# One core: a slot sort in two runs, a tile's x split by halves, and an expert loop turned by one step

## The chip, the cores and the metric

The kernel runs on one core of a Trainium2 chip. The metric is the device time of one execution in microseconds; lower is better. Matrix products run on TensorE (PE), elementwise work on VectorE (DVE) and ScalarE (ACT), indexed transfers are issued by GpSimd (POOL), the other transfers by SyncE (SP).

## What is computed

Three stages, each feeding the next:

```python
# 1: retention: state = gamma*state + k v^T ; y = scale * q state    (4 x 8 heads x 768 x 64)
# 2: dense, gated:
x = ((x @ w_a) * (x @ w_b)) @ w_out            # 3072 x 512, inner 1536
# 3: eight experts, one for each token:
logits = x @ w_gate
e_idx = np.argmax(logits, axis=1)
for e in range(8):
    mask = e_idx == e
    h = np.maximum(x[mask] @ w1[e], 0.0)       # 512 -> 1024
    out[mask] = gate_w[mask, None] * eom[mask, e, None] * (h @ w2[e])
```

The change touches only stage 3.

## The kernel before

Every factor of a large product is held as a high part and a remainder (`_hi`, `_lo`), and one product of 128 x 128 by 512 columns is three matrix products: hi*hi, hi*lo, lo*hi.

Stage 3 first sorts the 3072 tokens by expert into tiles of 128 slots, each tile of one expert. `pe_sort` (L1133) does it: 24 small products, one for each 128 tokens, sum `tile_hot` against `off_hot` into 34 columns of PSUM bank 7, which then hold the token number of each slot. `dve_route` (L1147) prepares those operands, waits for the sort (`slots_done`), writes `idx_gather`, builds the table of tiles (expert, run of the expert, whether new weights are needed here or next), and, further down in the same program, `hT_rest(dve, 1)`, the remainder of tile 1's transposed h. Tiles 0 and 1 are of expert 0 and are started before the sort is known.

A tile i passes these steps. POOL gathers its rows of x (`gather`, L1338). PE transposes them (`x_T`, L653, four transposes into bank 4); DVE splits them (`split_xe`, L665: hi, then lo). PE forms h (`up`, L1391, 24 products of 512 columns in two halves), ACT applies relu, PE transposes h (`h_T`, L1404, eight transposes), ACT copies the high part (`hT_part`, L1275), DVE forms the remainder (`hT_rest`, L1140). PE forms the output (`down`, L1412, eight steps k of three products), DVE scales it (`scale_y`, L1307), POOL scatters it to the output.

The order on each engine is that of its program. On PE a pair of tiles runs as h_T(2m), up(2m+1), x_T(2m+2), down(2m), h_T(2m+1), up(2m+2), x_T(2m+3), down(2m+1). A dictionary `between` puts other work ahead of a step k of a product. On DVE a tile runs as: weights of the next expert if needed, `split_xe(i+1)`, w2 if needed, `scale_y(i-1)`, `hT_rest(i)`.

The number of pairs depends on the data. `in_pairs` (L1227) runs a loop of fixed length and then a second one up to the possible maximum, in which each pass stands under a condition (L1232, L1233); PE, ACT, DVE and SP all run it. There are 27 tiles (0 to 26), so 13 pairs, of at most 16. Conditions and weight addresses come from registers that each engine's sequencer loads from the table. An engine's sequencer can be ahead of the engine. After the loops PE does h_T and down of the last tile (L1462, L1463), DVE its `scale_y`.

Of the kernel before, what the change touches and what calls it, by code (L numbers as in the profile page):

```python
# [4 lines left out]
F32 = mybir.dt.float32  # L5
# [7 lines left out]
P = 128  # L13
# [75 lines left out]
def build(nc, steps_in, weights_in, gates_in, w1_in, w2_in, const_in, xT_dram, x_dram, out):  # L89
# [31 lines left out]
    slot_scale = place("slot_scale", (P, COLS))  # L121

# [126 lines left out]
    yT_last = place("yT_last", (P, KD, GT))  # L249
    at[0] = common  # L250
# [396 lines left out]
    xe_T_done, xe_done = sem("xe_T_done"), sem("xe_done")  # L647
    scale_done, scale_out, scale_kept, rows_asked = sem("scale_done"), sem("scale_out"), sem("scale_kept"), sem("rows_asked")
# [16 lines left out]
    def split_xe(dve, i, s):  # L665
# [8 lines left out]
        if not (isinstance(i, int) and i < FIRST):  # L674
            keep_scale(i, xg[s])

# [456 lines left out]
    def pe_sort(pe):  # L1133
        pe.wait_ge(hot_done, 1)
        for t in range(TILES):
            ins = nc.tensor.matmul(bank[7][:, 0:COLS], off_hot[:, t, :], tile_hot[:, t],  # L1136
                                   start=(t == 0), stop=(t == TILES - 1))
        ins.then_inc(slots_done, 1)

    def hT_rest(dve, i):  # L1140
        for o in range(2):
            dve.wait_ge(hT_hi_done, 2 * i + o + 1)
            nc.vector.tensor_tensor(hT_lo[:, 4 * o:4 * o + 4].rearrange("p k t -> p (k t)"), bank[2 + o],  # L1143
                                    hT_hi[:, 4 * o:4 * o + 4].rearrange("p k t -> p (k t)").bitcast(F32),
                                    ALU.subtract).then_inc(hT_lo_done, 1)

    def dve_route(dve):  # L1147
# [65 lines left out]
        last = dve.value_load(n_pairs[0:1, 0:1], min_val=PAIRS_MIN, max_val=PAIRS_MAX)  # L1213
        v.tensor_copy(idx_last, idx_scatter[:, bass.ds(last * 2, 1)]).then_inc(scatter_ready, 1)
# [52 lines left out]
    def act_experts(act):  # L1267
# [7 lines left out]
        def hT_part(i):  # L1275
            for o in range(2):
                act.wait_ge(hT_done, 2 * i + o + 1)
                nc.scalar.copy(hT_hi[:, 4 * o:4 * o + 4].rearrange("p k t -> p (k t)"), bank[2 + o]).then_inc(hT_hi_done, 1)

        def tile(i):  # L1280
# [6 lines left out]
            hT_part(i)  # L1287

        def pair(m):
            tile(2 * m + 1)  # L1290
            tile(2 * m + 2)
# [12 lines left out]
        in_pairs(act, pairs, pair)  # L1304

    def dve_experts(dve):
# [5 lines left out]
        def tile(i, s):  # L1312
# [7 lines left out]
            hT_rest(dve, i)  # L1320

        def pair(m):
            tile(2 * m + 1, 1)
            tile(2 * m + 2, 0)

        split_xe(dve, 2, 0)
# [6 lines left out]
        in_pairs(dve, pairs, pair)  # L1333
        scale_y(pairs * 2, 0).then_inc(last_ye, 1)
# [51 lines left out]
    def pe_experts(pe):  # L1386
# [4 lines left out]
        def up(i, s, run, between=None):  # L1391
            half = (run % 2) * W1_SPAN
            pe.wait_ge(xe_done, 2 * i + 2)
# [18 lines left out]
        def down(i, s, run, between={}):  # L1412
            half = (run % 2) * W2_SPAN
# [122 lines left out]
```

## Time and profile before

| | |
|---|---|
| median of 3 runs | 1041.08 us (1039.38 to 1041.47) |
| profiled execution | 1042.53 us, its span 1040.7 us |
| mean granted TensorE clock | 0.995 |
| PE busy | 1018.0 us, 98% of the span |
| DVE busy | 554.4 us (53%) |
| ACT busy | 283.6 us (27%) |
| HBM traffic | 110 GB/s over the span |

How to read it: times in the trace count from the start of the span, in us, and durations marked ns in ns. A row of the chain of waits says what the end of the execution hung on at that time: an engine with its tile and line, or "issue", where nothing that the profile shows was waited for. A row of the timeline gives start, duration, engine, line, operation, output<-inputs and, in brackets, the engine's idle time before it and who ended it. A row of the table of stretches gives the stretch and its length, then for PE, PEld (weight loads), DVE, ACT and POOL the busy us with the count of instructions, then the granted clock of TensorE as a share of its full 2.4 GHz, the share of the DMA engines and GB/s. An engine's name with q is its sequencer. L1423 is a product of `down`, L1400 of `up`, L1408 a transpose of h, L659 one of x, L1136 a product of the sort.

### The profile page before, as it was taken

Reading aid. Unit: us, or ns where it says so; the run is one execution under the profiler, and the core shown is the slowest. Engines: PE = TensorE matmul, PEld = TensorE weight load, DVE = VectorE, ACT = ScalarE, POOL = GpSimd, SP = SyncE. Lnnn points to the kernel's source line nnn. Section 1 sums busy time; section 2 is a strip of 40 time slices with the busy share of each in tenths; the row PEclk is TensorE's granted clock in tenths of the full one; section 3 lists DMA queues with packets and bytes.
Section 4 is the critical chain, followed back from the end, with each engine's and each line's share of the span. In section 5 each row is a group of like instructions: output and inputs, shape, how many; then the busy total and the mean of one; then the engine's idle time right before and its main releaser. Section 6 shows DMA issues by size and latency. Waiting matters only on the chain.

```text
span 1040.7 us, 17289 instructions
## 1 busy us (share of the span) xinstructions
PE 1018.0 (98%) x5761; PEld 845.7 (81%) x5762; DVE 554.4 (53%) x1208; ACT 283.6 (27%) x490; POOL 112.4 (11%) x108
## 2 busy tenths in 40 slices
PE   6999999999999999999999999999999999999997
PEld 5887888888888888888888878887888888888886
DVE  3445333487557747773877223465454636354642
ACT  2534332221122122112211213130433424233431
POOL 4790000000000000000000000001111121111111
PEclk9999999999999999999999999998999999999999
DMA  9998800511061114103210212021744333344311
GB/s 362 363 293 268 219 1 1 140 53 47 5 152 51 41 30 134 51 31 84 88 51 21 82 41 81 1 61 34 290 146 170 121 128 131 118 155 162 118 36 37
DMA packets 53872, 114.48 MB, mean 110 GB/s; under 512 B 8749, under 2 KB 23405, under 8 KB 53296
## 3 DMA queue, kind: packets, MB, share of 16 engines
q1 hardware_dynamic: 48752, 98.95, 30.2%
q0 software_dynamic: 4480, 13.91, 3.9%
q8 instruction: 37, 0.61, 0.2%
q10 hardware_dynamic: 576, 0.79, 0.2%
q14 instruction: 27, 0.22, 0.1%
HBM read 96.81 MB, written 17.61 MB: 110 GB/s over the span
## 4 chain that ended last, share of the span: by engine, by line
PE 94%; DMA 3%; DVE 1%; issue 1%; ACT 1%; POOL 0%; ACTq 0%; DVEq 0%; POOLq 0%
PE bank L1061 38%; PE bank L1081 19%; PE bank L1423 14%; PE bank L1400 14%; PE bank L1408 2%; PE bank L601 2%; DMA rows<-in_steps 2%; PE bank L659 1%; PE bank L552 1%; PE bank L566 1%; DMA qdec_t<-in_consts 1%; PE bank L587 1%; PE bank L1136 0%; DVE hT_lo L1143 0%; PE bank L961 0%
## 5 line engine op out<-in xcount | busy, mean ns | idle before, releaser
L1061 PE MATMUL bank<-x_hi,wab_hi 128*128 128x512 f32 x576 | 224.4, 390 | 0.0
L1061 PE MATMUL bank<-x_hi,wab_lo 128*128 128x512 f32 x576 | 224.2, 389 | 0.0
L1061 PE MATMUL bank<-x_lo,wab_hi 128*128 128x512 f32 x576 | 224.1, 389 | 0.0
L983 DVE SCALAR_TENSOR_TENSOR products<-y_sb,gate_row 128x512 f32<-128x512 f32 x256 | 176.8, 691 | 22.8 <-DMA gate_row<-xT_dram 15.5
L1400 PE MATMUL bank<-w,xe 128*128 (+1 forms) x648 | 158.6, 399 | 0.5 <-DVE xe L671 0.5
L995 DVE TENSOR_TENSOR g_sb<-bank,b_sb 128x512 f32<-128x512 f32 x72 | 49.7, 690 | 175.0 <-PE bank L1061 175.0
L1400 PEld LDWEIGHTS bank<-w,xe 128*128 128x128 f32 x648 | 119.4, 188 | 28.1 <-issue 1.7
L1061 PEld LDWEIGHTS bank<-x_hi,wab_hi 128*128 128x128 f32 x576 | 108.1, 188 | 22.7 <-issue 0.2
L1061 PEld LDWEIGHTS bank<-x_hi,wab_lo 128*128 128x128 f32 x576 | 108.1, 188 | 22.5
L1061 PEld LDWEIGHTS bank<-x_lo,wab_hi 128*128 128x128 f32 x576 | 108.1, 188 | 22.3
L1081 PE MATMUL bank<-wo_hi,g_hi 128*128 128x512 f32 x288 | 113.3, 393 | 0.0
L1081 PE MATMUL bank<-wo_hi,g_lo 128*128 128x512 f32 x288 | 112.1, 389 | 0.0
L1081 PE MATMUL bank<-wo_lo,g_hi 128*128 128x512 f32 x288 | 112.1, 389 | 0.0
L773 ACT CAST g_hi<-g_sb 128x512 fp32r<-128x512 f32 x72 | 44.7, 621 | 231.7 <-DVE g_sb L995 231.7
L771 ACT COPY b_sb<-bank 128x512 f32<-128x512 f32 x72 | 42.3, 587 | 213.3 <-PE bank L1061 213.3
L1343 POOL DMA_INDIRECT xg<-x_rows,idx_gather x28 | 29.2, 1043 | 648.2 <-DVE idx_gather L953 597.2
L1423 PE MATMUL bank<-w_hi,hT_hi 128*128 (+1 forms) x216 | 88.0, 408 | 1.8 <-DVE hT_lo L1143 1.8
L1423 PE MATMUL bank<-w_hi,hT_lo 128*128 (+1 forms) x216 | 85.6, 396 | 0.0
L1423 PE MATMUL bank<-w_lo,hT_hi 128*128 (+1 forms) x216 | 85.5, 396 | 0.0
L997 DVE TENSOR_TENSOR g_lo<-g_sb,g_hi 128x512 fp32r<-128x512 f32 x72 | 49.9, 693 | 49.5 <-ACT g_hi L773 49.5
L1081 PEld LDWEIGHTS bank<-wo_hi,g_hi 128*128 128x128 f32 x288 | 54.1, 188 | 11.6 <-issue 0.8
L1081 PEld LDWEIGHTS bank<-wo_hi,g_lo 128*128 128x128 f32 x288 | 54.1, 188 | 11.4
(159 smaller groups left out, 1042.1 us busy)
## 6 DMA issues: line engine op xcount, KB each, us to landing
raw<-in_w SPq DMA_DIRECT2D x64, 512.0 KB, 5.9
gate_row<-xT_dram SPq DMA_DIRECT2D x64, 256.0 KB, 3.1
rows<-in_steps SPq DMA_DIRECT2D x20, 768.0 KB, 8.2
rows<-in_steps SPq DMA_DIRECT2D x24, 256.0 KB, 7.4
wab_raw<-in_weights SPq DMA_DIRECT2D x24, 256.0 KB, 9.3
x_rows<-y_sb SPq DMA_DIRECT2D x6, 1024.0 KB, 8.8
xT_dram<-x_all SPq DMA_DIRECT2D x4, 1024.0 KB, 12.8
x_raw<-xT_dram SPq DMA_DIRECT2D x16, 256.0 KB, 8.0
```

The source lines that it names most:

```text
L601: ins = nc.tensor.matmul(out_at(i, p, o), rows[:, c, 3, h * D:(h + 1) * D], probs[j][:, i, h, :], start=False, stop=(i == ROUND - 1 and p ...
L771: nc.scalar.copy(b_sb[:, f % 2], b_bank(f)).then_inc(b_read, 1)
L773: nc.scalar.copy(g_hi[:, f % 2], g_sb[:, f % 2]).then_inc(g_hi_done, 1)
L983: nc.vector.scalar_tensor_tensor(products, y_sb[:, t], 1.0, gate_row[e % GATE_SLOTS], ALU.mult, ALU.mult, accum_out=L3[:, t, e:e + 1]).the ...
L995: nc.vector.tensor_tensor(g_sb[:, f % 2], a_bank(f), b_sb[:, f % 2], ALU.mult).then_inc(g_done, 1)
L997: nc.vector.tensor_tensor(g_lo[:, f % 2], g_sb[:, f % 2], g_hi[:, f % 2].bitcast(F32), ALU.subtract).then_inc(g_lo_done, 1)
L1061: ins = nc.tensor.matmul(to, wab(w, f, j), x[s][:, k, :], start=(k == 0 and m == 0), stop=(k == KD - 1 and m == 2))
L1081: ins = nc.tensor.matmul(bank[4 + t], gp[:, f % 2, toks], wo(w, f), start=(f == 0 and m == 0), stop=(f == KF - 1 and m == 2))
L1343: nc.gpsimd.indirect_dma_start(out=xg_first[s] if i < FIRST else xg[s], out_offset=None, in_=x_rows[0:rows_there], in_offset=bass.Indirect ...
L1400: ins = nc.tensor.matmul(bank[o], x[:, s, k, :], w[:, bass.ds(half + (k * FE + o * 512), 512)], start=(k == 0 and m == 0), stop=(k == KD - ...
L1408: ins = nc.tensor.transpose(bank[2 + o][:, k * P:(k + 1) * P], h_sb[:, (4 * o + k) * P:(4 * o + k + 1) * P], ident)
L1423: ins = nc.tensor.matmul(bank[5 + s], h[:, k, :], w[:, bass.ds(half + k * DM, DM)], start=(k == 0 and m == 0), stop=(k == KE - 1 and m == 2))
```

## The change

1. `pe_sort` takes a half: twelve products each, in one accumulation. The first half stands ahead of step k=7 of tile 0's down product (all 24 stood ahead of k=6), the second behind tile 1's h transposes.
2. Of the two x transposes inside tile 1's down product, tile 2's stands ahead of k=7 (it was k=4), and tile 3's is moved into tile 2's up product, ahead of its step (0, 3). Tile 2's x is split by halves of its columns (`split_xe_early`, semaphore `xe_early`): hi and lo of the first half, then hi and lo of the rest; tile 2's up product starts with the first half and waits for the rest ahead of its step (0, 2).
3. The loop over pairs is turned by one step: on PE a pass now begins with the down product of the odd tile, and its first steps (`to_next_pair(0)`) stand ahead of the loop; on ACT and DVE `hT_part` and `hT_rest` of a tile move from the end of a tile to behind it, across the boundary of the loop.
4. The last tile's h transposes (all eight) stand ahead of k=5 of the down product before it. Its transposed h has tiles of its own (`hT_last`, in the room of raw1). PE waits for `scatter_ready` and loads `n_before`, the number of pairs less one, which DVE writes.

```diff
--- before.py
+++ after.py
@@ -119,6 +119,7 @@
     idx_gather = place("idx_gather", (P, COLS), I32)
     n_pairs = place("n_pairs", (P, 1), I32)
     slot_scale = place("slot_scale", (P, COLS))
+    n_before = place("n_before", (P, 1), I32)
 
     onehot = place("onehot", (P, TILES, NE))
     t_scale = place("t_scale", (P, TILES))
@@ -247,6 +248,8 @@
     at[0] = common
     part_last = place("part_last", (P, GT))
     yT_last = place("yT_last", (P, KD, GT))
+    at[0] = common
+    hT_last = tuple(place(f"hT_last_{n}", (P, KE, P), F32R) for n in ("hi", "lo"))
     at[0] = common
     base8 = place("base8", (P, TILES, NE))
     tile_eq = place("tile_eq", (P, TILES, COLS))
@@ -645,6 +648,7 @@
     gathered = [sem("gathered0"), sem("gathered1")]
     stored = [sem("stored0"), sem("stored1")]
     xe_T_done, xe_done = sem("xe_T_done"), sem("xe_done")
+    xe_early = sem("xe_early")
     scale_done, scale_out, scale_kept, rows_asked = sem("scale_done"), sem("scale_out"), sem("scale_kept"), sem("rows_asked")
     h_done, h_read, hT_done, hT_hi_done, hT_lo_done = sem("h_done"), sem("h_read"), sem("hT_done"), sem("hT_hi_done"), sem("hT_lo_done")
     ye_done, ye_read, ye_free, last_ye = sem("ye_done"), sem("ye_read"), sem("ye_free"), sem("last_ye")
@@ -673,6 +677,18 @@
         nc.vector.tensor_tensor(xe_lo[:, s], psum, xe_hi[:, s].bitcast(F32), ALU.subtract).then_inc(xe_done, 1)
         if not (isinstance(i, int) and i < FIRST):
             keep_scale(i, xg[s])
+
+    def split_xe_early(dve, i, s):
+        dve.wait_ge(xe_T_done, i + 1)
+        psum = bank[4].rearrange("p (k t) -> p k t", k=KD)
+        first, rest = slice(0, KD // 2), slice(KD // 2, KD)
+        nc.vector.tensor_copy(xe_hi[:, s, first], psum[:, first]).then_inc(xe_early, 1)
+        dve.wait_ge(xe_early, 1)
+        nc.vector.tensor_tensor(xe_lo[:, s, first], psum[:, first], xe_hi[:, s, first].bitcast(F32), ALU.subtract).then_inc(xe_early, 1)
+        nc.vector.tensor_copy(xe_hi[:, s, rest], psum[:, rest]).then_inc(xe_done, 1)
+        dve.wait_ge(xe_done, 2 * i + 1)
+        nc.vector.tensor_tensor(xe_lo[:, s, rest], psum[:, rest], xe_hi[:, s, rest].bitcast(F32), ALU.subtract).then_inc(xe_done, 1)
+        keep_scale(i, xg[s])
 
     def split_weight(eng, hi, run, raw, raw_in, w_hi_, w_lo_, span, hi_done, lo_done, parts):
 
@@ -1130,18 +1146,21 @@
         nc.tensor.matmul(bank[7][:, COUNT:COUNT + NE], ones_t, seen[:, TG, :], start=True, stop=True)
         pe_rank(pe, LAST)
 
-    def pe_sort(pe):
-        pe.wait_ge(hot_done, 1)
-        for t in range(TILES):
+    def pe_sort(pe, half):
+        if half == 0:
+            pe.wait_ge(hot_done, 1)
+        for t in range(half * TILES // 2, (half + 1) * TILES // 2):
             ins = nc.tensor.matmul(bank[7][:, 0:COLS], off_hot[:, t, :], tile_hot[:, t],
-                                   start=(t == 0), stop=(t == TILES - 1))
-        ins.then_inc(slots_done, 1)
-
-    def hT_rest(dve, i):
+                                   start=(t == 0), stop=(t == TILES - 1), skip_group_check=True)
+        if half == 1:
+            ins.then_inc(slots_done, 1)
+
+    def hT_rest(dve, i, hT=(hT_hi, hT_lo)):
+        high, low = hT
         for o in range(2):
             dve.wait_ge(hT_hi_done, 2 * i + o + 1)
-            nc.vector.tensor_tensor(hT_lo[:, 4 * o:4 * o + 4].rearrange("p k t -> p (k t)"), bank[2 + o],
-                                    hT_hi[:, 4 * o:4 * o + 4].rearrange("p k t -> p (k t)").bitcast(F32),
+            nc.vector.tensor_tensor(low[:, 4 * o:4 * o + 4].rearrange("p k t -> p (k t)"), bank[2 + o],
+                                    high[:, 4 * o:4 * o + 4].rearrange("p k t -> p (k t)").bitcast(F32),
                                     ALU.subtract).then_inc(hT_lo_done, 1)
 
     def dve_route(dve):
@@ -1211,6 +1230,7 @@
         link(v.tensor_tensor(inv_s, inv_s, inv_e, ALU.add))
         link(v.tensor_copy(idx_scatter, inv_s))
         last = dve.value_load(n_pairs[0:1, 0:1], min_val=PAIRS_MIN, max_val=PAIRS_MAX)
+        v.tensor_scalar(n_before, n_pairs, -1, None, ALU.add)
         v.tensor_copy(idx_last, idx_scatter[:, bass.ds(last * 2, 1)]).then_inc(scatter_ready, 1)
 
 
@@ -1272,10 +1292,10 @@
                     act.wait_ge(hT_done, 2 * i - 1 + o)
                 nc.scalar.activation(h_sb[:, o * 512:(o + 1) * 512], bank[o], ACT.Relu).then_inc(h_read, 1)
 
-        def hT_part(i):
+        def hT_part(i, high=hT_hi):
             for o in range(2):
                 act.wait_ge(hT_done, 2 * i + o + 1)
-                nc.scalar.copy(hT_hi[:, 4 * o:4 * o + 4].rearrange("p k t -> p (k t)"), bank[2 + o]).then_inc(hT_hi_done, 1)
+                nc.scalar.copy(high[:, 4 * o:4 * o + 4].rearrange("p k t -> p (k t)"), bank[2 + o]).then_inc(hT_hi_done, 1)
 
         def tile(i):
             with act.If(entry(act, i, NEW_NEXT) == 1):
@@ -1284,10 +1304,11 @@
             relu(i, False)
             with act.If(entry(act, i, NEW_HERE) == 1):
                 split_w2(act, True, entry(act, i, RUN))
-            hT_part(i)
 
         def pair(m):
+            hT_part(2 * m)
             tile(2 * m + 1)
+            hT_part(2 * m + 1)
             tile(2 * m + 2)
 
         split_w2(act, True, 0, (3,))
@@ -1302,6 +1323,7 @@
             split_w1(act, True, 1)
         tile(2)
         in_pairs(act, pairs, pair)
+        hT_part(pairs * 2, hT_last[0])
 
     def dve_experts(dve):
         def scale_y(i, s):
@@ -1317,13 +1339,14 @@
             with dve.If(entry(dve, i, NEW_HERE) == 1):
                 split_w2(dve, False, entry(dve, i, RUN))
             scale_y(i - 1, 1 - s).then_inc(ye_read, 1)
-            hT_rest(dve, i)
 
         def pair(m):
+            hT_rest(dve, 2 * m)
             tile(2 * m + 1, 1)
+            hT_rest(dve, 2 * m + 1)
             tile(2 * m + 2, 0)
 
-        split_xe(dve, 2, 0)
+        split_xe_early(dve, 2, 0)
         split_xe(dve, 3, 1)
         with dve.If(entry(dve, 1, NEW_NEXT) == 1):
             split_w1(dve, False, 1)
@@ -1331,6 +1354,7 @@
         tile(2, 0)
         pairs = dve.value_load(n_pairs[0:1, 0:1], min_val=PAIRS_MIN, max_val=PAIRS_MAX)
         in_pairs(dve, pairs, pair)
+        hT_rest(dve, pairs * 2, hT_last)
         scale_y(pairs * 2, 0).then_inc(last_ye, 1)
 
 
@@ -1388,9 +1412,12 @@
         pe.sem_inc(ye_free, 2)
 
 
-        def up(i, s, run, between=None):
+        def up(i, s, run, between=None, early=None):
             half = (run % 2) * W1_SPAN
-            pe.wait_ge(xe_done, 2 * i + 2)
+            if early is None:
+                pe.wait_ge(xe_done, 2 * i + 2)
+            else:
+                pe.wait_ge(early, 2)
             pe.wait_ge(w1_lo_done, run * PARTS + PARTS)
             for o in range(2):
                 for k in range(KD):
@@ -1409,8 +1436,9 @@
                 ins.then_inc(hT_done, 1)
 
 
-        def down(i, s, run, between={}):
+        def down(i, s, run, between={}, hT=(hT_hi, hT_lo)):
             half = (run % 2) * W2_SPAN
+            high, low = hT
             pe.wait_ge(hT_lo_done, 2 * i + 1)
             pe.wait_ge(w2_lo_done, run * PARTS + PARTS)
             pe.wait_ge(ye_read, i - 1 + 2)
@@ -1419,30 +1447,34 @@
                     between[k]()
                 if k == KE // 2:
                     pe.wait_ge(hT_lo_done, 2 * i + 2)
-                for m, (h, w) in enumerate(((hT_hi, w2_hi), (hT_hi, w2_lo), (hT_lo, w2_hi))):
+                for m, (h, w) in enumerate(((high, w2_hi), (high, w2_lo), (low, w2_hi))):
                     ins = nc.tensor.matmul(bank[5 + s], h[:, k, :], w[:, bass.ds(half + k * DM, DM)],
                                            start=(k == 0 and m == 0), stop=(k == KE - 1 and m == 2))
             ins.then_inc(ye_done, 1)
 
 
-        run_even, run_odd = pe.alloc_register("run_even"), pe.alloc_register("run_odd")
+        run_before, run_even, run_odd = (pe.alloc_register(f"run_{n}") for n in ("before", "even", "odd"))
 
         def run_of(register):
             return pe.snap(register, min_val=0, max_val=NE - 1)
 
-        def pair(m):
-            even, odd = run_of(run_even), run_of(run_odd)
-            h_T(2 * m)
-            up(2 * m + 1, 1, odd)
-            x_T(pe, 2 * m + 2, 0, m + 1, bank[4])
-            down(2 * m, 0, even)
-            even = entry(pe, 2 * m + 2, RUN)
+        def to_next_pair(n, even, odd):
+            h_T(2 * n + 2)
+            up(2 * n + 3, 1, odd)
+            x_T(pe, 2 * n + 4, 0, n + 2, bank[4])
+            down(2 * n + 2, 0, even)
+            pe.reg_mov(run_before, odd)
+            even = entry(pe, 2 * n + 4, RUN)
             pe.reg_mov(run_even, even)
-            pe.reg_load(run_odd, tile_tab[0:1, bass.ds(2 * m + 3, 1), RUN])
-            h_T(2 * m + 1)
-            up(2 * m + 2, 0, even)
-            x_T(pe, 2 * m + 3, 1, m + 1, bank[4])
-            down(2 * m + 1, 1, odd)
+            pe.reg_load(run_odd, tile_tab[0:1, bass.ds(2 * n + 5, 1), RUN])
+            h_T(2 * n + 3)
+            up(2 * n + 4, 0, even)
+            x_T(pe, 2 * n + 5, 1, n + 2, bank[4])
+
+        def pair(n):
+            before, even, odd = run_of(run_before), run_of(run_even), run_of(run_odd)
+            down(2 * n + 1, 1, before)
+            to_next_pair(n, even, odd)
 
 
         pe.wait_ge(g_done, GROUPS * KF + 2)
@@ -1451,16 +1483,25 @@
         pe_logits(pe, LAST, part_last)
         pe.wait_ge(h_read, 2)
         up(1, 1, 0, {(1, 0): lambda: h_T(0), (1, 1): lambda: pe_counts(pe)})
-        down(0, 0, 0, {KE - 2: lambda: pe_sort(pe)})
+        down(0, 0, 0, {KE - 1: lambda: pe_sort(pe, 0)})
         h_T(1)
-        down(1, 1, 0, {KE // 2: lambda: x_T(pe, 2, 0, 1, bank[4]), KE - 1: lambda: x_T(pe, 3, 1, 1, bank[4])})
+        pe_sort(pe, 1)
+        down(1, 1, 0, {KE - 1: lambda: x_T(pe, 2, 0, 1, bank[4])})
         pairs = pairs_of(pe)
         pe.reg_load(run_even, tile_tab[0:1, 2:3, RUN])
         pe.reg_load(run_odd, tile_tab[0:1, 3:4, RUN])
-        up(2, 0, run_of(run_even))
-        in_pairs(pe, pairs, pair)
-        h_T(pairs * 2)
-        down(pairs * 2, 0, run_of(run_even))
+        even, odd = run_of(run_even), run_of(run_odd)
+        up(2, 0, even, {(0, 2): lambda: pe.wait_ge(xe_done, 2 * 2 + 2), (0, 3): lambda: x_T(pe, 3, 1, 1, bank[4])}, xe_early)
+        to_next_pair(0, even, odd)
+        with pe.Fori(1, PAIRS_MIN - 1) as n:
+            pair(n)
+        with pe.Fori(PAIRS_MIN - 1, PAIRS_MAX - 1) as n:
+            with pe.If(pairs > n + 1):
+                pair(n)
+        pe.wait_ge(scatter_ready, 1)
+        n = pe.value_load(n_before[0:1, 0:1], min_val=PAIRS_MIN - 1, max_val=PAIRS_MAX - 1)
+        down(2 * n + 1, 1, run_of(run_before), {KE // 2 + 1: lambda: h_T(2 * n + 2)})
+        down(2 * n + 2, 0, run_of(run_even), {}, hT_last)
 
     with nc.Block(no_gpsimd_drain=True) as block:
```

## Rows read from the trace of the kernel before

**Rows 1.** The page, part 4: shares of the chain that ended last, by engine.

```profile
PE 94%; DMA 3%; DVE 1%; issue 1%; ACT 1%; POOL 0%; ACTq 0%; DVEq 0%; POOLq 0%
```

**Rows 2.** Table of stretches: us, busy us by engine (count), clock, DMA, GB/s.

```profile
706.90:709.39 2.49, 2.30 (x20) 2.14 (x20) 1.58 (x6) 0.00 (x0) 0.00 (x0) 1.00 0.00 0
709.39:715.64 6.25, 5.71 (x22) 4.62 (x21) 2.68 (x13) 1.10 (x2) 2.00 (x2) 0.50 0.24 70
715.64:719.63 3.99, 3.99 (x9) 3.13 (x10) 1.40 (x6) 0.07 (x1) 0.00 (x0) 0.50 0.08 27
719.63:724.62 4.99, 4.54 (x24) 3.42 (x23) 2.52 (x5) 0.00 (x0) 1.00 (x1) 1.00 0.00 0
```

**Rows 3.** Chain of waits from 706 to 725 us: start us, us, what.

```profile
706.19 1.02 DVE tile_hot L1183
...
707.25 3.38 PE bank L1136 x24
710.64 2.75 PE bank L1423 x6
...
714.89 0.70 DVE hT_lo L1143
...
715.64 4.88 PE bank L1423 x12
...
723.51 0.70 DVE xe L671
...
724.62 5.87 PE bank L1400 x24
```

**Rows 4.** Chain of waits, one steady tile: down product, then the transposes.

```profile
737.85 5.48 PE bank L1423 x24
743.33 0.87 PE bank L1408 x8
```

**Rows 5.** Timeline of DVE around the tile table: start us, us, line, operands, wait.

```profile
708.13 0.45 DVE L1189 TENSOR_TENSOR tl<-tl,e 128x280 f32<-128x280 f32 x1
710.75 0.19 DVE L1192 TENSOR_SCALAR idx_gather<-bank 128x32 int32<-128x32 f32 x1 [2.16 <-PE bank L1136]
...
712.57 0.27 DVE L1206 CAST tile_tab<-inv 128x34 int32<-128x34 f32 x1
```

**Rows 6.** Timeline of POOL, the gather of tile 2; and its time to landing.

```profile
711.78 1.00 POOL L1343 DMA_INDIRECT xg<-x_rows,idx_gather  x1 [34.26 <-DVE idx_gather L1192]
...
DMA to landing us min/median/max: 3.3/3.4/3.4
```

**Rows 7.** Chain of waits at the last two tiles.

```profile
1028.00 0.45 PE bank L1408 x4
...
1029.09 0.70 DVE hT_lo L1143
...
1029.79 0.37 issue
1030.16 5.74 PE bank L1423 x24
```

**Rows 8.** Timeline of DVE at the last two tiles: tile 25's scale.

```profile
1028.13 0.75 DVE L1310 TENSOR_SCALAR ye<-bank,slot_scale 128x512 f32<-128x512 f32 x1 [4.09 <-PE bank L1423]
```

**Rows 9.** Sequencers at L1232 after 1021 us: ns, first and last start; a load.

```profile
L1232 PEldq ALU_OP  x4: 32/36/36, 1023.8 to 1026.0; - x4
L1232 DVEq ALU_OP  x4: 40/40/40, 1029.6 to 1031.7; - x4
L1232 DVEq COMPARE_BRANCH  x4: 50/56/66, 1029.7 to 1031.7; - x4
...
L1225 PEldq TENSOR_LOAD <-n_pairs x1: 491/491/491, 722.6 to 722.6; - x1
```

**Rows 10.** The page's clock in 40 slices; PE's waits (us, times, longest).

```profile
PEclk9999999999999999999999999998999999999999
...
PE bank L566 <- issue: 2.2, 2, 1.4
```

## The prediction

> **What bounds the kernel.** The page's chain is read first: TensorE (PE) carries 94% of it [rows 1]. An edit pays only where PE waits, or where it works slower than it could. The granted clock, read next in a table of stretches, shows the second: it stands at 1.00 up to 709.39 us, at 0.50 from there to 719.63 (1.2 of 2.4 GHz), at 1.00 afterwards [rows 2]. Before the fall PE had ended a dense product, waited a little, and worked on the sort, whose products are 34 columns wide. The chain of waits then names what lies in that stretch [rows 3]: the sort (707.25), the last six products of tile 0's down product, tile 1's h transposes, a wait for DVE's hT_lo (714.89), tile 1's down product (715.64), DVE's xe (723.51), and the up product of tile 2 (724.62). From there to 1028 us PE has no gap: a tile repeats one pattern, 24 down products in 5.48 us and 8 transposes in 0.87 [rows 4]. Last comes the end of the chain: between the down products of tiles 25 and 26 PE stands for most of 2.16 us [rows 7]. So there are two places to win, 706.9 to 724.6 and 1028.0 to 1030.2.
>
> Prices at full clock: a wide product 5.48/24 = 0.228 us, 8 transposes 0.87 and 4 of them 0.44 [rows 4]; a sort product 0.115 (of the sort's 3.38 us 2.14 lie ahead of the fall and 1.24 behind it, where each costs double: (2.14 + 0.62)/24) [rows 2, 3], half a sort 1.38. At half clock a wide product costs 0.44 (nine in 3.99) [rows 2]; tile 0's last six took 2.75 [rows 3].
>
> **Sort in two runs.** Before, the product k=6 could have started at 706.90, where the first stretch of [rows 2] begins, but the sort stood ahead of it and waited for tile_hot (706.19 + 1.02 = 707.21) [rows 3]. In the new order three products go first: 706.90 to 707.58. Nothing waits now. First half of the sort to 708.96, k=7 to 709.64, eight transposes to 710.51, second half to 711.89. I take full clock up to here, since three wide products now interrupt the sort. slots_done thus comes at 711.89, 1.25 us later than before (710.64).
>
> What is late next is DVE. Its program is unchanged here: it waits for slots_done, writes idx_gather and the tile table, and only then takes tile 1's hT_rest. Before, idx_gather started at 710.75 and the last table operations at 712.57 [rows 5]; a DVE free for the next at about 712.80 waited until 714.89 for the transposes, which came after. Now the transposes are long done and the table is what hT_rest stands behind: idx_gather 712.00, hT_lo 714.05 to 714.75, first product of down(1) at 714.79. PE stands still from 711.89 to 714.79, 2.90 us, where it stood 0.55 before. The start of down(1) moves by only 715.64 - 714.79 = 0.85 us.
>
> The transfers that slots_done starts move too. The gather of tile 2 was issued at 711.78 and landed 3.4 us later [rows 6]; now 713.03 and 716.4. Its transposes come after 21 products, at 719.58 or later, so it is covered by 3 us; the gather for tile 3 (1.3 us behind) is covered too, its transposes now lie inside up(2). SyncE's load of the next expert waits for gather 4, which waits for tile 2's scale; that comes no later than now.
>
> **The clock** is what I can't read off directly. If it stays up: 21 products end at 719.58, four transposes at 720.02. If it falls in the new stall and comes back at 719.63 as it did before: 4.84 us at 0.44 are 11 products, the other 10 take 2.28, the transposes end at 722.35, 2.3 us later. If it stays low through all 21: 724.03 + 0.44, another 2.1 us. I take the middle one. For a fall speaks that before, 2.14 us of narrow products and a short wait ended in one [rows 2, 3], and now 0.87 of transposes, 1.38 of narrow products and 2.90 of nothing stand together. Against it speaks that PE had idle times of up to 1.4 us during the attention without losing the clock [rows 10]; the new idle time is twice that. The Trainium skill ("TensorE: Matmul & The Clock Gate", HAM oscillation) says that PE that waits between bursts of matmuls falls back to the half clock; the fall behind the sort agrees in kind, and by that rule the new stall has to lose the clock, which is my middle case.
>
> **Tile 3 after, x of tile 2 by halves.** After, up(2) needs tile 2's first half only. DVE takes 0.70 for 512 columns [rows 3] and 0.45 for 280 [rows 5], so 0.43 for 256: hi and lo of the first half 0.02 + 0.43 + 0.02 + 0.43 = 0.90. Then 0.41 in which PE's queue resolves its registers (724.62 - 723.51 - 0.70) [rows 3]; I keep it. up(2) starts 1.31 us after the transposes: 721.3 with full clock, 723.7 in the middle case, against 724.62. The second half is ready 0.9 us later, while six products cover 1.36. Tile 3's transposes (0.44) lay before up(2) and now lie inside it. So up(2) ends 724.62 - 723.66 - 0.44 = 0.5 us earlier in the middle case, 2.9 earlier with full clock, 1.6 later if the clock stays low throughout.
>
> **The loop turned by one step.** PE's order in the steady tiles is the same; only the jump back moves from behind the down product to in front of it, at one register move more. DVE and ACT have their jump before hT instead of after. A jump is a few tenths [rows 9] and DVE waits there anyway. I cost it at nothing; the cover is PE's sequencer, which issued the end of down(25) at 1023.8 while the array ended it at 1028.00 [rows 7, 9], 4.2 us ahead.
>
> **The last tile.** Its transposes go behind k=4 of down(25), and ACT's copy is hidden there. But DVE's program puts scale_y(25) ahead of hT_rest(26), and scale_y waits for down(25) to end. So: down(25) ends at 1028.00 + 0.87 = 1028.87; scale_y starts 0.13 later (1028.13 - 1028.00) [rows 7, 8], 1029.00. Between it and hT_rest(26) now lie the jump back and the three passes of the conditional loop that do nothing (27 tiles, 13 pairs of at most 16). Before, DVE's sequencer ran them in the shade of down(26): its loop additions stand at 1029.6 and 1031.7, four of them, 0.7 us a pass, 2.15 us to the end of the last [rows 9]. Set behind scale_y's issue they end at 1031.2; hT_lo (0.70) starts about 1031.25, ends 1031.95, PE starts 0.37 later [rows 7], at 1032.3 instead of 1030.16: **2.2 us later**. At best, if the passes hid wholly behind scale_y's 0.75 [rows 8], it is 1029.75 + 0.70 + 0.37 = 1030.8, still 0.7 later. At worst PE's own sequencer is late too: its passes (1023.8 to 1026.0 and a last branch, 2.5 us) and the new load of n_before (0.49 for such a load [rows 9], with register work behind it some 0.8, an estimate) make 3.3 us against a lead that, counted in queued instructions with four short transposes among them, is some 3.6; I take 0 and bound it at 0.5 above. The Trainium skill ("Advanced Engine Details and Errata", Control Flow Timing) gives about 108 ns for a compare-and-branch; six of them in three passes would be 0.65 us, hidden behind scale_y, and the tail would be 0.7 later instead of 2.2. The rows' 0.7 us a pass decides for me; that rule is rival two.
>
> **Sum** against the profiled execution (span 1040.7, with 1.8 around it): -0.5 + 2.2 = +1.7 us. That execution is 1.45 us over the median of the runs; I put the difference on the median: 1041.08 + 1.7 = **1042.8 us**. Its own range: the fall's end moves it by about 0.9 either way.
>
> **Rivals.** One: the clock stays at 1.00 through the stall. -2.9 + 2.2 = -0.7, 1040.4 us. Two: the empty passes cost what the branches' recorded durations say (0.04 to 0.06 us each on DVE [rows 9]) and hide behind scale_y: -0.5 + 0.7 = +0.2, 1041.3; together with rival one -2.2, 1038.9, the only way to a faster kernel that I find. Three, the slower side: the clock comes back only with the dense products after the stall, when most of down(1) is through: +1.6 + 2.2 = +3.8, 1044.9 us. It decides against me when the clock is back later than about 720.5 in the time of this trace. The change not doing what it says (the sort's two halves as costly together, or no fall avoided within the sort) is in the middle case already: the fall would only come 2 us earlier, and cost 0.6 more.
>
> **Chances.** Forecast 0.47, rival one 0.17, rival two 0.10, both together 0.10, rival three 0.16. Bounds for what this measurement can tell from no change are 0.2%, 2.1 us: faster is under 1039.0, slower over 1043.2. Faster: the 0.10 of both together and a little of rival one, 0.14. Slower: rival three and the upper end of the forecast, 0.30. The rest, 0.56, is within. The range leaves out little of rival three and the both-case: 1039.2 to 1044.7.
>
> **What would show it.** In the profile after: the sort in two groups with no wait for tile_hot; a PE wait of 2.9 us ahead of tile 1's down product, released by DVE hT_lo; a stretch of clock 0.50 that begins in or near it; up(2) about 1.3 us behind tile 2's transposes; steady tiles as before, 12.4 us each; and between the last two down products about 3.4 us, with scale_y, the loop's branches on DVE's queue, and then hT_lo. A kernel faster by over 2 us would mean that DVE reached hT_rest(1) or hT_rest(26) earlier than its program order says.

## The result and the profile after

The changed kernel took 1047.98 us in the median (1045.67 to 1048.88, 5 executions) against 1039.38 (1038.5 to 1041.47, 5 executions) before: ratio 1.0075, 95% interval 1.0056 to 1.0094. The forecast was 1042.8, in a range up to 1044.7. The change is slower, and by much more than forecast. Over more executions of both kernels (79 of the kernel before, 11 of the changed one, below) the means are 1040.87 and 1047.49 us, a difference of 6.6; this is the figure that the sums below are held against. Three executions that stood far off (one of e1_front at 1138.76 us with a clock of 0.85, two of the kernel before at 1275.81 and 2073.73 us) are left out of every number of this document.

The profiled execution of the changed kernel has a span of 1045.0 us, 4.3 more than that of before; in it PE was busy 1017.6 us (1018.0 before). First the chain of waits from the end of tile 0's down product to the up product of tile 2, which answers to [rows 3]. L1153 is the sort, L1451 `down`, L1435 h's transposes, L663 x's, L1427 `up`:

```profile
708.75 1.25 PE bank L1153 x12
710.00 0.79 PE bank L1451 x3
710.79 0.87 PE bank L1435 x8
711.66 1.26 PE bank L1153 x12
...
713.02 0.19 DVE idx_gather L1211
...
715.10 0.51 DVE hT_lo L1162
...
715.66 6.64 PE bank L1451 x21
722.30 0.45 PE bank L663 x4
...
722.77 0.43 DVE xe L685
...
723.23 0.43 DVE xe L687
723.67 0.30 issue
723.97 2.37 PE bank L1427 x9
```

The sort stands in two groups of 1.25 us (0.104 a product). Between the end of the second (712.92) and tile 1's down product (715.66) PE does nothing; DVE writes idx_gather and the tile table and only then forms hT_lo. Up(2) follows its transposes after 1.22 us: DVE's hi and lo of the first half, 0.43 each, and 0.30 in which nothing that the profile shows was waited for. Then the down product itself: 21 products in 6.64 us, not the 4.8 that they cost at full clock (21 times 0.228). The table of stretches (us; busy PE, PEld, DVE, ACT, POOL; clock; DMA; GB/s) says why, and shows the same thing again at the end, ahead of and in down(26):

```profile
712.92:715.66 2.74, 0.00 (x1) 0.00 (x1) 2.54 (x14) 0.00 (x0) 1.30 (x2) 1.00 0.00 0
715.66:719.00 3.34, 3.34 (x9) 2.62 (x10) 1.38 (x7) 0.00 (x0) 0.69 (x1) 0.57 0.56 161
719.00:722.30 3.30, 3.30 (x16) 2.69 (x15) 0.00 (x0) 0.00 (x0) 0.00 (x0) 0.92 0.00 1
1029.23:1032.77 3.54, 0.00 (x1) 0.01 (x1) 1.82 (x3) 0.00 (x0) 1.00 (x1) 1.00 0.09 35
1032.77:1036.50 3.73, 3.73 (x10) 2.94 (x11) 0.21 (x1) 0.00 (x0) 0.00 (x0) 0.61 0.10 37
1036.50:1040.13 3.63, 3.61 (x15) 2.60 (x13) 0.00 (x0) 0.00 (x0) 0.00 (x0) 0.93 0.00 0
```

Both waits, 2.74 and 3.54 us with PE at 0.00 busy, end before the clock falls; in this execution it falls just behind each, on the dense products. In a second profiled execution of the same kernel (a2_after) it fell inside the first wait, 0.9 us after PE had stopped at 711.78, and the 21 products behind took longer:

```profile
714.52 7.41 PE bank L1451 x21
```

The end of the chain, against [rows 7]:

```profile
1026.26 0.87 PE bank L1435 x8
1027.14 2.10 PE bank L1451 x9
...
1029.35 0.06 DVE ye L1332
1029.41 0.03 issue
1029.44 0.06 DVEq L1252
1029.50 0.24 issue
...
1031.59 0.06 DVEq L1161
1031.65 0.05 issue
1031.70 0.70 DVE hT_last_lo L1162
1032.40 0.37 issue
1032.77 7.36 PE bank L1451 x24
```

Rows DVEq are DVE's sequencer: L1252 is the conditional loop's line. From 1029.44 to 1031.59 it runs the jump and the three empty passes, 2.15 us as read off [rows 9], between tile 25's scale and hT_last_lo. Down(26) then takes 7.36 us, 5.74 before [rows 7]. The steady tiles are unchanged to within 0.01 us each: PE is in one unbroken chain from 731.62 to 1022.10, and a down product takes 5.46 to 5.50 us, as in [rows 4].

### The profile page after: what moved, and what is told of

Read it like the earlier page. It is cut to its first block, busy times and chain, and to the rows that moved or that the text cites. A ratio compares the mean times of both kernels' runs of the same rounds, so it can differ in the third digit from the quotient of the medians.

```text
span 1045.0 us, 17350 instructions
## 1 busy us (share of the span) xinstructions
PE 1017.6 (97%) x5761; PEld 844.9 (81%) x5762; DVE 554.5 (53%) x1211; ACT 283.6 (27%) x490; POOL 112.4 (11%) x108
## 4 chain that ended last, share of the span: by engine, by line
PE 96%; DMA 2%; issue 1%; DVE 1%; ACT 0%; POOL 0%; ACTq 0%; DVEq 0%; POOLq 0%
PE bank L1077 38%; PE bank L1097 19%; PE bank L1427 15%; PE bank L1451 14%; PE bank L1435 2%; PE bank L604 2%; PE bank L555 2%; PE bank L663 1%; PE bank L569 1%; PE bank L590 1%; DMA rows<-in_steps 1%; DMA qdec_t<-in_consts 1%; PE bank L1153 0%; PE bank L977 0%; PE bank L844 0%
## 5 line engine op out<-in xcount | busy, mean ns | idle before, releaser
L1427 PE MATMUL bank<-w,xe 128*128 (+1 forms) x648 | 158.9, 399 | 0.5 <-DVE xe L687 0.5
L1427 PEld LDWEIGHTS bank<-w,xe 128*128 128x128 f32 x648 | 119.3, 188 | 28.2 <-issue 1.8
L1451 PE MATMUL bank<-w_hi,hT_hi 128*128 (+1 forms) x208 | 84.3, 405 | 2.8 <-DVE hT_lo L1162 2.8
L1451 PE MATMUL bank<-w_hi,hT_lo 128*128 (+1 forms) x208 | 82.0, 394 | 0.0
L1451 PE MATMUL bank<-w_lo,hT_hi 128*128 (+1 forms) x208 | 81.6, 393 | 0.0
```

The lines of the kernel that those rows point to most:

```text
L1427: ins = nc.tensor.matmul(bank[o], x[:, s, k, :], w[:, bass.ds(half + (k * FE + o * 512), 512)], start=(k == 0 and m == 0), stop=(k == KD - ...
L1451: ins = nc.tensor.matmul(bank[5 + s], h[:, k, :], w[:, bass.ds(half + k * DM, DM)], start=(k == 0 and m == 0), stop=(k == KE - 1 and m == 2))
```

## The experiments

All ran with the kernel before beside them; the ratio is to that. Clock is the mean over a kernel's executions of each one's mean granted clock. A mean clock of 0.995 in a span of 1040 us stands for some 10 us at 1.2 GHz, and costs about 5 us; so span x (1 - clock) is an estimate of what the clock took. It is a rough one: a profile gives the clock to three digits, and it counts the low clock behind PE's last product too, which costs nothing. In e10_mid_fixed's profile that is the only one: 1.00 up to 1033.20 us, PE's last product ending at 1031.05, and 0.53 behind it. So 0.6 or 0.7 us in the last column stand for no loss.

| kernel | executions | median us | ratio to before, 95% | clock | clock's cost, us |
|---|---|---|---|---|---|
| b0_before | 12 | 1040.82 | 1.0005 (0.9993 to 1.0017) | 0.9979 | 2.2 |
| a2_after | 6 | 1047.09 | 1.0061 (1.0046 to 1.0076) | 0.9948 | 5.4 |
| e1_front (parts 1, 2) | 11 | 1043.42 | 1.0028 (1.0016 to 1.0040) | 0.9969 | 3.2 |
| e8_sort_only (part 1) | 12 | 1042.53 | 1.0015 (1.0005 to 1.0025) | 0.9969 | 3.2 |
| e9_x_only (part 2) | 12 | 1040.29 | 0.9992 (0.9979 to 1.0004) | 0.9980 | 2.1 |
| e2_tail (parts 3, 4) | 6 | 1045.61 | 1.0045 (1.0028 to 1.0062) | 0.9967 | 3.5 |
| e3_dve_ahead | 12 | 1042.68 | 1.0018 (1.0007 to 1.0029) | 0.9975 | 2.6 |
| e4_tail_fixed | 12 | 1041.24 | 1.0007 (0.9994 to 1.0019) | 0.9969 | 3.2 |
| e6_fill_mid | 6 | 1045.87 | 1.0049 (1.0032 to 1.0066) | 0.9968 | 3.3 |
| e7_fill_both | 12 | 1043.55 | 1.0026 (1.0014 to 1.0037) | 0.9993 | 0.7 |
| e5_both | 12 | 1036.83 | 0.9967 (0.9955 to 0.9979) | 0.9993 | 0.7 |
| e10_mid_fixed | 5 | 1037.52 | 0.9963 (0.9949 to 0.9976) | 0.9994 | 0.6 |

**The kernels themselves.** Theory A: the new waits cost their own length and, beyond it, the clock. Theory B: something else, such as the turned loop.

> The kernel before, unchanged, to see span and granted clock of each of its executions. Its profiled execution had 10.2 us at half clock behind the sort, mean 0.995. Theory A (what the change costs beyond its waits is TensorE's clock): the shorter executions of this kernel, near 1038.5 us, hold the clock longer than the profiled one, mean 0.997 or more, and the longer ones, near 1041.5, about 0.995. Theory B (the clock has no part in the difference): all executions stand at 0.995 and their spans differ for another reason.

Measured: over the 79 executions of the kernel before that ran beside the experiments, 20 had a clock of 1.000 and took 1039.05 us in the mean; the 29 at 0.998 took 1041.1, the 8 at 0.995 took 1043.3. So in a quarter of its executions the kernel before loses nothing, and the profiled execution on which the forecast rests, 1042.53 us at 0.995, is among its slowest. Another profiled execution of the same kernel has the low clock for 3.4 us, not 10.2:

```profile
706.00:710.02 4.02, 3.83 (x28) 3.25 (x26) 2.88 (x7) 0.00 (x0) 0.00 (x0) 1.00 0.00 0
710.02:713.43 3.41, 3.41 (x11) 2.74 (x11) 1.99 (x12) 0.00 (x0) 1.08 (x2) 0.50 0.00 0
713.43:722.54 9.11, 7.70 (x42) 6.01 (x40) 4.53 (x12) 1.07 (x2) 1.92 (x2) 1.00 0.21 59
```

The size and the duration of the fall belong to the execution, not to the code alone. Theory A holds for the difference of some 4 us between the ends. It had the clock of the executions near 1041.5 us too low (0.996 to 0.998, not 0.995), and the clock is not all of the spread: those at 1.000 lie between 1037.89 and 1040.7 us. What takes the clock of the kernel before behind its sort was not tested: both its profiles show the fall there, and PE waits no longer than 0.2 us ahead of it.

> The changed kernel again, for more executions on the chip of the other runs. Theory (clock costs and waits add): its mean is the 1040.8 of the kernel before, plus 2.4 (parts 1 and 2, e1_front) plus 4.4 (parts 3 and 4, e2_tail): 1047.5; half of that excess goes with a mean clock of 0.994 to 0.996 against 0.998. If it came out under 1045, the first five executions were a poor sample.

Measured: 1047.09 median, 1047.40 mean, 6.5 us above the 1040.87 of the kernel before. Parts 1 and 2 (+2.3 in the means, e1_front) and parts 3 and 4 (+4.3, e2_tail) add up to it. Its clock cost is 5.4 us against 2.2: 3.2 of the 6.5 us are clock, the rest is waits.

**Which part.** e1_front has only the edits of parts 1 and 2, e2_tail only those of parts 3 and 4. In e2_tail the sort's call reads, against the changed kernel (the x edits are taken back too),

```diff
-        down(0, 0, 0, {KE - 1: lambda: pe_sort(pe, 0)})
+        down(0, 0, 0, {KE - 2: lambda: (pe_sort(pe, 0), pe_sort(pe, 1))})
         h_T(1)
-        pe_sort(pe, 1)
```

> Parts 1 and 2 of the change alone (sort in two runs, x of tile 2 by halves), loop and last tile as before. Theory A: PE waits 2.7 us for DVE ahead of tile 1's down product, the clock falls in or behind that wait; against the kernel before about +1 us (0 to +3), some 1040.5. Theory B (the two parts do what they are meant to, the loss lies wholly in the loop and the last tile): about 1 to 3 us faster than before, 1037 to 1038.

> Parts 3 and 4 of the change alone (loop turned, last tile's transposes inside the down product before it); sort and x transposes where they were. Theory A: between the last two down products PE waits 3.5 us for DVE, which has to scale tile 25 and run its empty loop passes first; the gap costs 2.2 to 2.6 us, and the clock that falls in it 0 to 1.7 more: +2.4 to +4.5, 1042 to 1044. Theory B (a cost of the turned loop itself, spread over the 24 tiles): the steady tiles are longer than 12.38 us, and the total is +7 or more.

Measured: e1_front 1043.42, at the upper end of theory A's band and not below the kernel before, as theory B had it. e2_tail 1045.61 (mean 1045.12), above A's 1042 to 1044 and below B's +7; it shows A's picture, a PE wait of 3.5 us for hT_last_lo and a last down product that is slow in the same way (chain of waits):

```profile
1026.79 2.10 PE bank L1451 x9
...
1032.42 7.36 PE bank L1451 x24
```

Its steady down and up products are 5.49 and 5.60 us, so B's cost spread over the tiles is not there. Against the mean of the kernel before it is +4.3, inside A's +2.4 to +4.5; only the absolute time is above the forecast.

**Part 1 or part 2.** e8_sort_only leaves the x transposes where they were; e9_x_only leaves the sort in one run, has tile 3's transposes and the wait for the second half inside tile 2's up product, and

```diff
-        down(1, 1, 0, {KE // 2: lambda: x_T(pe, 2, 0, 1, bank[4]), KE - 1: lambda: x_T(pe, 3, 1, 1, bank[4])})
+        down(1, 1, 0, {KE - 1: lambda: x_T(pe, 2, 0, 1, bank[4])})
```

> Only the sort in two runs; x of tiles 2 and 3 as before. Theory (the sort's second half behind the h transposes makes DVE build the tile table while PE waits, and that is the cost of parts 1 and 2): the 2.75 us wait is there as in e1_front, the time is that of e1_front, 1043.2 within 0.5. Rival (the moved x transposes cost it): near the kernel before, 1041.

> Only x of tile 2 by halves and tile 3's transposes inside the up product of tile 2; sort in one run as before. Theory: the gap ahead of that up product stays near 0.5 us, the transposes only change place; 0 to 0.5 us faster than the kernel before, 1040.5. Rival (it carries the loss of e1_front): 1043.

Measured: the sort alone is slower than before, its interval clear of 1, by 1.8 us in the means (1042.65), a little less than the 1043.2 within 0.5 that I expected; the x halves alone (1040.28) are not told from no change. The two add up to +1.2 where e1_front has +2.3; with executions that scatter over 4 to 5 us, whether the parts add or act together stays open. PE's waits of e8_sort_only (us, times, longest) name the one of 2.8 us behind the sort; the other of the two is the last tile's, which before has too:

```profile
PE bank L1425 <- DVE hT_lo L1145: 4.0, 2, 2.8
PE bank L1402 <- DVE xe L671: 0.4, 1, 0.4
```

**The wait ahead of tile 1's down product.** e3_dve_ahead is the changed kernel with one line moved on DVE:

```diff
+        hT_rest(dve, 1)
         dve.wait_ge(slots_done, 1)
         v.tensor_scalar(idx_gather[:, FIRST:], bank[7][:, FIRST:COLS], -1.0, 0.0, ALU.add, ALU.max).then_inc(gather_ready, 1)
...
-        hT_rest(dve, 1)
         v.tensor_scalar(inv_e, inv, 0.0, float(2 * NT), ALU.is_equal, ALU.mult)
```

> The changed kernel with one thing moved: DVE forms the remainder of tile 1's h ahead of its wait for the sort, not behind the tile table. Theory A: PE's wait of 2.75 us ahead of tile 1's down product shrinks to under 0.3 us, and without it the clock holds; against the changed kernel (1048) 2.7 us for the wait plus 1.5 to 3.5 for the clock: 1042 to 1044. Rival (the narrow products of the sort pull the clock down, the wait does not matter): only the wait is won, 1045, and the half clock stays behind the sort.

Measured: 1042.68, in the means 4.8 us under the changed kernel. The wait is gone: the second half of the sort ends at 713.33 and the 21 products begin there and take 4.90 us (chain of waits), with the clock at 1.00 behind the same narrow products:

```profile
712.08 1.25 PE bank L1153 x12
713.33 4.90 PE bank L1451 x21
718.23 0.53 PE bank L663 x4
```

```profile
711.21:713.33 2.12, 2.12 (x22) 2.12 (x20) 0.96 (x2) 1.07 (x2) 0.00 (x0) 1.00 0.00 0
713.33:720.18 6.85, 6.12 (x30) 4.58 (x29) 4.30 (x23) 0.00 (x0) 1.99 (x2) 1.00 0.28 79
1025.30:1028.83 3.53, 0.00 (x1) 0.01 (x1) 1.82 (x3) 0.00 (x0) 1.00 (x1) 1.00 0.09 35
1028.83:1036.20 7.37, 7.33 (x24) 5.58 (x24) 0.21 (x1) 0.00 (x0) 0.00 (x0) 0.77 0.05 19
```

The last two rows are the tail of that kernel, untouched: an empty 3.53 us, then a low clock. The rival, that the narrow products take the clock, falls for this order of the work.

**Is it the emptiness of the wait?** e6_fill_mid keeps the wait and fills it with work whose result nobody reads; e7_fill_both does so at the end too (14 products into bank 0).

```diff
         pe_sort(pe, 1)
+        for _ in range(11):
+            nc.tensor.matmul(bank[6], xe_hi[:, 1, 0, :], w1_hi[:, 0:512], start=True, stop=True)
```

> The changed kernel with 11 wide products more (results unused) behind the second half of the sort, 2.5 us of PE work inside the 2.75 us that PE waits there for DVE. The wait's end does not move. Theory (it is the empty wait that takes the clock, and the clock that costs beyond it): the clock holds in this stretch, tile 1's down product runs at 0.228 us a product at once: 1.6 to 3 us faster than the changed kernel although more work is done, some 1045.5. Rival (the clock falls by the narrow products or by chance in time): no gain, 1048 or later.

> As e6_fill_mid, and 14 wide products more (results unused), 3.2 us of PE work, inside the 3.5 us wait between the last two down products. Theory: the last down product takes 5.7 us instead of up to 7.4; 1.6 us faster than e6_fill_mid, some 1044, and no execution under a mean clock of 0.999. Rival: same as e6_fill_mid.

Measured: with more work on PE the kernel is faster, by 1.9 us and then by another 2.1 (means 1047.5 over the eleven executions of the changed kernel, 1045.6 and 1043.5). In e6_fill_mid's table of stretches and chain the clock stands at 1.00 from the sort on, and the 21 products take 5.08 us where they took 6.64:

```profile
712.33:716.32 3.99, 3.90 (x23) 3.06 (x22) 2.54 (x14) 0.67 (x2) 1.30 (x2) 1.00 0.01 4
716.32:723.07 6.75, 6.22 (x28) 4.82 (x29) 2.54 (x10) 0.00 (x0) 0.70 (x1) 1.00 0.28 78
```

```profile
716.32 5.08 PE bank L1451 x21
```

In e7_fill_both the 14 unused products (L1507) fill the last wait, which keeps its length (1027.53 to 1031.09), and the down product behind them takes 5.74 us, the value of [rows 7]:

```profile
1027.53 3.27 PE bank L1507 x14
...
1031.09 5.74 PE bank L1451 x24
```

Its executions have clocks of 0.998 to 1.000, one at 0.998; I had expected none under 0.999. This shows theory A directly: DVE's work that ends the waits did not change, PE got more to do, and 4 us came back. It also prices the waits alone. e7_fill_both still lies 0.26% above the kernel before, but that one has a lower clock; between executions with a clock of 1.000 (5 of e7_fill_both, mean 1043.10, and the 20 of the kernel before, 1039.05) it is some 4 us.

**The tail, with DVE's order mended.** e4_tail_fixed lets the scale of an odd tile cross the loop's boundary:

```diff
-            scale_y(i - 1, 1 - s).then_inc(ye_read, 1)
+            if s == 1:
+                scale_y(i - 1, 1 - s).then_inc(ye_read, 1)
         def pair(m):
             hT_rest(dve, 2 * m)
+            scale_y(2 * m - 1, 1).then_inc(ye_read, 1)
             tile(2 * m + 1, 1)
...
         hT_rest(dve, pairs * 2, hT_last)
+        scale_y(pairs * 2 - 1, 1).then_inc(ye_read, 1)
```

> The changed kernel with DVE's order altered at the loop's boundary: the scale of an odd tile comes behind the h remainder of the even tile after it, so the last tile's remainder waits neither for tile 25's scale nor, exposed, for the empty passes. Theory (the tail costs its gap and the clock that falls in it): the 3.5 us gap between the last two down products goes, the last down product takes 5.7 us instead of 7.36: about 5 us faster than the changed kernel (1048), near 1043, and about 1.3 under e1_front (1043.5). Rival (the gap only moves, for instance to a wait for ye_free or for PE's own queue): under 2 us won.

> Both repairs in one: tile 1's h remainder ahead of DVE's wait for the sort, and the scale of the odd tile behind the even tile's remainder. Theory: no PE wait over 0.7 us is left from the sort to the end, the clock falls in few executions or none; e3_dve_ahead (1042.7) less the 5 us of the tail: 1037.5, faster than the kernel before (1040.7) by 0.3%. Rival: the two gains overlap and it stays within 0.2% of the kernel before.

> Parts 1 and 2 with DVE's remainder of tile 1's h ahead of its wait for the sort; loop and last tile as before. Theory: the wait goes and the clock holds: e5_both (1036.8) plus the gap that its last tile no longer has (2.16 less 0.87 us): 1038.2, 2.5 under the kernel before. Rival (e5's gain is owed to the tail): 1040 or more.

Measured: e4_tail_fixed 1041.24, 6 us under the changed kernel in the means, more than expected. The wait ahead of tile 1's down product is still there, and in its profile the clock fell inside it, near 715.1, with the wait ending at 716.07; the 21 products behind it took 7.78 us, at a mean clock of 0.63. e5_both, which has e3's line too, 1036.83: faster than the kernel before, interval 0.9955 to 0.9979. Ten of its twelve executions have a clock of 0.999 or 1.000, and all five of e10_mid_fixed, against 21 of 79 of the kernel before: with no wait behind it, the sort in two runs does keep the clock. The profiled execution of e5_both is its slowest, 1040.74 us, and lost the clock in stage 1, which the change does not touch and the prediction calls the attention (0.55 from 33.50 to 36.80 us, 0.64 from 80.10 to 84.90, behind PE waits of 1.96 and 1.78 us); from 700 to 1034 us it is at 1.00. In that profile the last 33 products run in one piece from behind the h transposes, across both down products, and of PE's waits only the one for x and relu's are left:

```profile
1025.66 0.87 PE bank L1438 x8
1026.54 7.54 PE bank L1454 x33
```

```profile
PE bank L1430 <- DVE xe L687: 0.6, 1, 0.6
PE bank L1438 <- ACT h_sb L1293: 0.2, 1, 0.2
```

e10_mid_fixed has the sort and the x halves with DVE's line ahead, and the tail of before, with its 1.3 us wait:

```profile
PE bank L1441 <- DVE hT_lo L1158: 1.3, 1, 1.3
PE bank L1418 <- DVE xe L684: 0.6, 1, 0.6
```

It took 1037.52, mean 1037.45, against a mean of 1037.40 for e5_both. The 1.3 us that the mended tail should be worth beyond it is not seen in the means, but e5_both's holds two executions that lost the clock elsewhere; without them it is 1036.8. The traces, both at 1.00 in this stretch, show 0.9 us: from the start of the sort to the end of the last down product 322.47 us in e10_mid_fixed (708.58 to 1031.05) and 321.57 in e5_both (712.51 to 1034.08). That is one profile each, and e10_mid_fixed ran only five times. That the gain of e5_both over the kernel before comes mainly from the middle does follow.

## Why the prediction was wrong

- **Waits and their lengths: right.** PE's wait ahead of down(1): 2.90 us forecast, 2.74 measured. From the start of tile 0's k=6 to that of down(1): 7.89 forecast (706.90 to 714.79), 7.59 measured (708.07, three products ahead of the sort, to 715.66). Up(2) behind the transposes: 1.31 forecast, 1.22 measured. Between the last two down products 3.4 forecast, 3.54 measured; the empty passes 2.15 and 2.15. Steady tiles unchanged, PE's sequencer in time, no gather late: right.
- **Where the miss lies.** In the means the change costs 6.6 us where +1.7 was forecast. Of the 4.9 us between them 2.1 lie in the tail's term (+2.2 forecast, +4.3 in e2_tail) and 2.8 in the middle's (-0.5 forecast, +2.3 in e1_front). The waits were right; both terms were mis-sized by the clock, in two ways.
- **The tail's sum: the step that failed.** The clock behind the tail's wait was left at nothing. "At 1032.3 instead of 1030.16: 2.2 us later" was the whole price of the tail. The clock was weighed for the wait of 2.9 us and not for the one of 3.4 in the same text. The down product behind it took 7.36 us for 5.74, 1.6 us more, and e7_fill_both won 2.1 in the means by filling that wait. Tile 26's transposes, the wait and its down product together are 0.87 + 3.54 + 7.36 = 11.77 us in the changed kernel's profile and 2.16 + 5.74 = 7.90 before [rows 7]: +3.9, not +2.2.
- **The middle's sum: the second term, mis-sized by its base.** The forecast of -0.5 compared the change with the one profiled execution of before, in which the clock was low for 10.2 us [rows 2], and I carried that difference over to the median. From the time at which tile 0's k=6 could start to the end of tile 2's up product, that execution took 23.59 us (706.90 to 730.49), the one of b0_before 21.06 (707.34 to 728.40) and the changed kernel 22.23 (708.07 to 730.30), where 23.1 was forecast. So the stage itself came out 0.9 us better than forecast, better than in the one reference and worse than in the other. The kernel before has in the mean 0.998, a cost of 2.2 us, and in a quarter of its executions none, while the changed one costs 5.4 to 5.9 of clock in its mean, and none of its eleven executions is above 0.996. At full clock on both sides the old order was better placed than I had written down: its sort in one run would end near 710.0 (707.25 and 24 times 0.115), and behind it 6 products, 4 transposes, ACT's copy (0.59 in the chain of b0_before) and hT_lo come to about 1.37 + 0.44 + 0.02 + 0.59 + 0.02 + 0.70, so down(1) would start near 713.2, 1.6 us ahead of the new order (an estimate, from [rows 3, 4] and that chain). With the fall in the reference this did not show.
- **The clock in the new stall: right in kind.** That it would fall with 2.9 us of nothing behind transposes and narrow products was the forecast's middle case, and e3_dve_ahead and e6_fill_mid show both ways round that the empty wait is what does it. The Trainium skill's rule ("TensorE: Matmul & The Clock Gate", HAM oscillation), that PE waiting between bursts of matmuls falls back, agrees with four profiled waits here (2.7 and 3.5 us in the changed kernel, 3.5 in e2_tail and in e3_dve_ahead), each with the low clock right behind it. The length of a wait does not settle it here: in a2_after and e4_tail_fixed the clock fell inside the wait of 2.74 us, and at one place in stage 1 a wait of 1.8 us has the low clock behind it in e5_both and not in the changed kernel's profile.
- **Rival two (empty passes hidden)** is refuted: 2.15 us on the chain. The figure of "Advanced Engine Details and Errata", Control Flow Timing, in the Trainium skill (about 108 ns a compare-and-branch) is above the 50 to 66 ns recorded for one on DVE [rows 9], and yet a pass costs 0.69 us: rows of "issue" of 0.21 to 0.24 us lie behind each jump (1029.50 in the chain above).
- **Rival three** had the direction and a size (+3.8) nearer than the forecast's, but not the way: the clock was back well within down(1) (0.57 from 715.66 to 719.00, 0.92 from there to 722.30), as in the forecast's middle case. That its number comes near is luck. The chances put 0.30 on slower; the range ended at 1044.7, under even rival three's own 1044.9, and 3.3 us (0.3%) under the result.

## What to carry to other kernels

A wait on TensorE is worth its length and the clock behind it: here waits of 2.7 and 3.5 us cost some 2 us more each in the means (1.9 and 2.1 won by filling them), on products that came after them. When work is moved on one engine, read the program of the engine that it hands over to: here DVE stood with the right operand ready behind a table (2.1 us) and behind a scale and three empty loop passes (2.15 us), and two such moves on DVE, with nothing changed on PE, turned +0.6% into a gain of 0.3% (e5_both). Before a difference is taken against a profiled execution, ask whether its clock is typical of the kernel.

## What the runs showed of the hardware

- Whether and how long the clock falls differs between executions of one kernel: 10.2 us at half clock in one profile of the kernel before, 3.4 in another, 1.000 as the mean of the span in 20 of 79 executions.
- In the changed kernel's profile the clock fell after the wait had ended, on dense products: PE idle 712.92 to 715.66, low behind it (0.57 in the mean from 715.66 to 719.00); idle 1029.23 to 1032.77, low behind it. In a2_after and e4_tail_fixed it fell inside the wait of 2.74 us, 0.9 and 1.7 us after PE had stopped, and the 21 products behind took 7.41 and 7.78 us.
- One pass of a loop that does nothing costs DVE's sequencer 0.69 us, 0.42 of it in rows of "issue" behind its two jumps, although its recorded instructions last 0.04 to 0.07 us each.
- 1.25 us of narrow products, behind eight transposes and followed at once by dense ones, kept the clock at 1.00 in the profiles of e3_dve_ahead, e5_both and e10_mid_fixed.
